# Fused attention and two feed-forward layers on one core: the first group's keys and values laid four tokens deep over 128 partitions

## What is computed

```
kv  = einsum('bhsd,bhse->bhde', k, v)          # 64 x 64 per head, a sum over 576 tokens
out = einsum('bhsd,bhde->bhse', q, kv)
x   = out / sqrt(mean(out*out, -1) + 1e-6) * g_norm   -> (2304, 512)
x   = silu(x @ w_in) @ w_out                    # layer 1, d_ff 2048
y   = ((x @ w_a) * (x @ w_b)) @ w_out2          # layer 2, d_ff 1536
```

## Time and profile before

| | |
|---|---|
| median of 3 runs | 872.2 us (870.73 to 873.78) |
| the profiled execution | 873.04 us |
| its span, first to last instruction | 871.2 us |
| mean granted TensorE clock | 0.998 |
| TensorE matmul busy | 860.4 us, 99% of the span |
| VectorE, ScalarE, GpSimd busy | 510.6, 279.0, 610.1 us |
| moved by DMA | 55.56 MB, mean 64 GB/s |

### The profile page before, as it was taken

One profiled execution on the slowest core, in us unless ns is written; L12 is line 12 of the kernel. 1 busy time (PEld: TensorE's weight loads), 2 busy tenths in 40 slices (PEclk: granted clock), 3 DMA queues, 4 the chain that ended last, 5 costly groups with the idle time before them and its releaser, 6 DMA issues.

```text
span 871.2 us, 16097 instructions
## 1 busy us (share of the span) xinstructions
PE 860.4 (99%) x6208; PEld 813.8 (93%) x6208; DVE 510.6 (59%) x776; ACT 279.0 (32%) x465; POOL 610.1 (70%) x889
## 2 busy tenths in 40 slices
PE   8899999999999999999999999999999999999998
PEld 5699999999999999999999999999999999999997
DVE  4665656757886666665765355364484553544636
ACT  3764434534543323222532122121242211212210
POOL 2566545666578777766778697797889876877760
PEclk9999999999999999999999999999999999999999
DMA  9664123111011111111101111021011330210104
GB/s 300 158 156 106 49 57 75 50 49 49 26 49 49 46 28 50 50 49 49 49 25 49 50 49 49 25 63 60 25 49 49 109 98 25 74 49 25 49 25 109
DMA packets 47002, 55.56 MB, mean 64 GB/s; under 512 B 11728, under 2 KB 32464, under 8 KB 46928
## 3 DMA queue, kind: packets, MB, share of 16 engines
q1 hardware_dynamic: 44192, 49.55, 19.9%
q10 hardware_dynamic: 2736, 4.98, 1.8%
HBM read 49.81 MB, written 4.72 MB: 63 GB/s over the span
## 4 chain that ended last, share of the span: by engine, by line
PE 98%; DVE 1%; issue 1%; ACT 0%; POOL 0%; POOLq 0%
PE ps L777 49%; PE ps L863 8%; PE ps L864 8%; PE ps L865 8%; PE ps L885 6%; PE ps L887 6%; PE ps L886 6%; PE ps L794 3%; PE ps L737 2%; PE ps L747 1%; PE ps L989 1%; PE ps L709 1%; PE ps L723 1%; DVE o_sb L1350 0%; DVE stat L1331 0%
## 5 line engine op out<-in xcount | busy, mean ns | idle before, releaser
L777 PE MATMUL ps<-x_hi,w_hi 128*128 128x288 f32 x1064 | 229.8, 297 | 0.5 <-issue 0.3
L777 PE MATMUL ps<-x_lo,w_hi 128*128 128x288 f32 x1064 | 228.1, 296 | 0.0
L777 PE MATMUL ps<-x_hi,w_lo 128*128 128x288 f32 x1064 | 226.8, 295 | 0.0
L777 PEld LDWEIGHTS ps<-x_hi,w_hi 128*128 128x128 f32 x1064 | 179.0, 188 | 13.7 <-issue 5.1
L777 PEld LDWEIGHTS ps<-x_hi,w_lo 128*128 128x128 f32 x1064 | 171.7, 189 | 0.0
L777 PEld LDWEIGHTS ps<-x_lo,w_hi 128*128 128x128 f32 x1064 | 169.9, 188 | 0.0
L1142 ACT COPY kept<-ps 128x576 f32<-128x576 f32 x114 | 73.2, 642 | 288.1 <-PE ps L777 287.6
L523 POOL TENSOR_SCALAR w_hi<-wt 128x256 fp32r<-128x256 f32 x152 | 69.9, 460 | 123.4 <-PE ps L777 116.4
L1473 DVE TENSOR_TENSOR xy<-xy,ps 128x384 f32<-128x384 f32 (+1 forms) x188 | 94.0, 510 | 89.0 <-PE ps L865 88.7
L863 PE MATMUL ps<-g_hi,d_hi 128*128 128x384 f32 x384 | 129.0, 336 | 0.2
L864 PE MATMUL ps<-g_lo,d_hi 128*128 128x384 f32 x384 | 128.9, 336 | 0.0
(11 more groups left out here) (111 smaller groups left out, 1236.7 us busy)
## 6 DMA issues: line engine op xcount, KB each, us to landing
raw<-in_moe_w_out_dram SPq DMA_DIRECT2D x28, 512.0 KB, 3.6
raw<-in_moe_w_in_dram SPq DMA_DIRECT2D x15, 512.0 KB, 3.5
raw<-in_moe_w_a_dram SPq DMA_DIRECT2D x12, 512.0 KB, 3.5
raw<-in_moe_w_b_dram SPq DMA_DIRECT2D x12, 512.0 KB, 3.5
kvq<-in_k_dram SPq DMA_DIRECT2D x8, 576.0 KB, 5.5
out_dram<-xy SPq DMA_DIRECT2D x26, 128.0 KB, 2.4
kvq<-in_v_dram ACTq DMA_DIRECT2D x4, 576.0 KB, 11.4
kvq<-in_v_dram SPq DMA_DIRECT2D x4, 576.0 KB, 5.9
```

The source lines that it names most:

```text
L777: mm = pe.matmul(ps[:, bank + s, 0:PART], w, x[:, n, c, s * PART:(s + 1) * PART], start=(begins and first), stop=last, skip_group_check=no ...
```

## The change

- Group 0's k and v: tokens 0 to 511 of a head are spread over all 128 partitions, four tokens deep (`main_heads`, one load for each batch: 256 pieces of 1 KB), and the last 64 tokens go, for the two heads, on 64 partitions each (`rest_heads`, one load for each head of k and of v: 128 pieces of 256 bytes). `kv(0, h)` is then 16 matmuls of 128 rows and 4 of 64 rows, where it was 36 of 64 rows.
- SyncE issues k, all rests and all of q; ScalarE issues v alone. SyncE also waits for the fourth `kv` before it loads group 1.
- Warm-up: 26 matmuls of 56 columns and 8 of 48, for 3 and 2 of 512.
- One order for all head pairs of group 0: `o_turn` of the pair before goes in turn with `q_kv`, and VectorE interleaves normalising and `qT_keep` from h = 0 on.
- Group 1's `kv_keep` copies first the bank that TensorE needs next and frees it with a semaphore of its own (`kv_first`).
- The last rest of segments 2 and 3 goes from GpSimd to VectorE (one instruction).
- The second half of the last down tile goes to `BANK_A`.

```diff
-    POOL_RESTS = (((0, 0), (0, 1), (7, 0), (7, 1), (5, 0), (5, 1)), (6,))
+    POOL_RESTS = (((0, 0), (0, 1), (7, 0), (7, 1), (5, 0), (5, 1)), (6,), (), ())
...
-    WARM = (3, 2)
+    WARM = ((26, 56), (8, 48))
...
+        def main_heads(h, which, bb):
+
+            dst = kvq[h][:, which, main_at(bb, 0, 0).start:main_at(bb, 1, DEEP - 1).stop].rearrange("p (h e) -> p h e", h=2)
+            return dst, (k, v)[which][bb, 2 * h:2 * h + 2, 0:MAIN].rearrange("h (p t) d -> p h (t d)", t=DEEP)
+
+        def rest_heads(h, which, odd):
+            dst = kvq[h][odd * HALF:(odd + 1) * HALF, which, rest_at(0).start:rest_at(1).stop]
+            return dst.rearrange("p (b d) -> p b d", b=2), (k, v)[which][0:2, 2 * h + odd, MAIN:].rearrange("b p d -> p b d")
...
-            return BANK_D + (tile_turn[DOWN0[-1] - 1] + c) % 2
+            return (tile_bank(DOWN0[-1] - 1), BANK_A)[c]
...
             for h in range(PAIRS):
-                sp.dma_start(*heads(0, h, 0)).then_inc(kv_in[h], 16)
-                sp.dma_start(*queries(h, 0)).then_inc(q_in[h], 16)
+                for bb in range(2):
+                    sp.dma_start(*main_heads(h, 0, bb)).then_inc(kv_in[h], 16)
+                for which in range(2):
+                    for odd in range(2):
+                        sp.dma_start(*rest_heads(h, which, odd)).then_inc(kv_in[h], 16)
+                for bb in range(2):
+                    sp.dma_start(*queries(h, bb)).then_inc(q_in[h], 16)
...
             sp.wait_ge(q_in[PAIRS - 1], 32)
+            sp.wait_ge(kv_mm, PAIRS)
             load_heads(0)
...
-                if u == PROD0[seg_of(pair_of(u))]:
-                    x_rest(seg_of(pair_of(u)), 6)
+                if u == PROD0[1]:
+                    x_rest(1, 6)
...
+                    for t in range(DEEP):
+                        for odd, bank in enumerate((b0, b1)):
+                            for bb in range(2):
+                                cols = main_at(bb, odd, t)
+                                pe.matmul(ps[bb * HALF:(bb + 1) * HALF, bank, 0:HD],
+                                          kvq[h][:, 0, cols], kvq[h][:, 1, cols], start=(t == 0), stop=False)
...
+                if G:
+                    turn[BANK_D + kv_order(G, h)[0]] = (kv_first, h + 1)
...
                 for j in range(JS):
-                    if h > 1:
+                    if h:
                         o_turn(0, h - 1, j, result_bank(h - 1, j))
                     q_kv(0, h, j, prod_bank(h, j))
...
             for h in range(PAIRS):
-                nc.scalar.dma_start(*heads(0, h, 1)).then_inc(kv_in[h], 16)
-                nc.scalar.dma_start(*queries(h, 1)).then_inc(q_in[h], 16)
+                for bb in range(2):
+                    nc.scalar.dma_start(*main_heads(h, 1, bb)).then_inc(kv_in[h], 16)
...
-                flush(3, 4)
+                flush(3, 3)
+                late_rest(pp, 6)
+                flush(4, 4)
```

More of the change, by code:

```diff
@@ L30, in fused_attention_ffn_kernel @@
     TILE3 = 3 * P
+    DEEP = SEQ // P
+    MAIN = DEEP * P
     JS = ROWS // 3
     UNITS = PAIRS * JS
-    assert KT == 4 and ROWS % 3 == 0 and SEQ == 2 * PART and PART <= 512
+    assert KT == 4 and ROWS % 3 == 0 and SEQ == 2 * PART and PART <= 512 and SEQ - MAIN == HALF
     SEGS = [(g, layer) for layer in (1, 2) for g in range(GROUPS)]
@@ L398, in x_split @@
         def x_split(seg, n, c=1):
[L400 to L405, removed]
+            what = n if seg else (n, c)
+            split, signal = (POOL_RESTS, side_ready) if what in POOL_RESTS[seg] else (DVE_RESTS, x_ready)
+            return signal, split[seg].index(what) + 1 + sum(len(rests) for rests in split[:seg])
         def temps(seg):
@@ L467, in load_heads @@
                 for which in range(2):
-                    sp.dma_start(*heads(1, h, which)).then_inc(kv_in[0], 16)
+                    sp.dma_start(*heads(h, which)).then_inc(kv_in[0], 16)
                 for bb in range(2):
@@ L703, in kv @@
                 wait_turn(b1)
-                for t in range(ROWS):
+                if G:
+                    for t in range(ROWS):
+                        for odd, bank in enumerate((b0, b1)):
+                            rows = slice(odd * HALF, odd * HALF + HD)
+                            for bb in range(2):
+                                cols = slice(bb * SEQ + t * HD, bb * SEQ + (t + 1) * HD)
+                                mm = pe.matmul(ps[bb * HALF:(bb + 1) * HALF, bank, 0:HD],
+                                               kvq[0][rows, 0, cols], kvq[0][rows, 1, cols],
+                                               start=(t == 0), stop=(t == ROWS - 1))
+                else:
+                    for t in range(DEEP):
+                        for odd, bank in enumerate((b0, b1)):
+                            for bb in range(2):
+                                cols = main_at(bb, odd, t)
+                                pe.matmul(ps[bb * HALF:(bb + 1) * HALF, bank, 0:HD],
+                                          kvq[h][:, 0, cols], kvq[h][:, 1, cols], start=(t == 0), stop=False)
                     for odd, bank in enumerate((b0, b1)):
-                        rows = slice(odd * HALF, odd * HALF + HD)
                         for bb in range(2):
-                            cols = slice(bb * SEQ + t * HD, bb * SEQ + (t + 1) * HD)
+                            rows, cols = slice(odd * HALF, (odd + 1) * HALF), rest_at(bb)
                             mm = pe.matmul(ps[bb * HALF:(bb + 1) * HALF, bank, 0:HD],
-                                           kvq[buf][rows, 0, cols], kvq[buf][rows, 1, cols],
-                                           start=(t == 0), stop=(t == ROWS - 1))
+                                           kvq[h][rows, 0, cols], kvq[h][rows, 1, cols], start=False, stop=True)
                 mm.then_inc(kv_mm, 1)
                 turn[b0] = turn[b1] = (kv_kept, PAIRS * G + h + 1)
+                if G:
+                    turn[BANK_D + kv_order(G, h)[0]] = (kv_first, h + 1)
             def q_turn(G, h, j, bank):
@@ L983, in layer2, with warm @@
                 down2(pp - 1, 8)
-            def warm(count):
+            def warm(count, cols):
                 for _ in range(count):
                     zeros = wt[:, 0:2, :].rearrange("p a n -> p (a n)")
-                    pe.matmul(ps[:, first_bank(1, 0), :], ident[:], zeros, start=True, stop=True)
+                    pe.matmul(ps[:, first_bank(1, 0), 0:cols], ident[:], zeros[:, 0:cols], start=True, stop=True)
             pe.wait_ge(consts, 3)
             pe.wait_ge(cleared, 1)
-            warm(WARM[0])
+            warm(*WARM[0])
             kv(0, 0)
-            warm(WARM[1])
+            warm(*WARM[1])
             for j in range(JS):
@@ L1070, in kv_keep @@
                 act.wait_ge(cleared, 2)
-                for odd, bank in enumerate((BANK_D, BANK_D + 1)):
+                for place, odd in enumerate(kv_order(G, h)):
                     if n == 0 and odd:
@@ L1076, in kv_keep @@
                     for bb in range(2):
-                        cp = nc.scalar.copy(kv_sb[rows, h % 2, bb, rows], ps[bb * HALF:(bb + 1) * HALF, bank, 0:HD])
+                        cp = nc.scalar.copy(kv_sb[rows, h % 2, bb, rows],
+                                            ps[bb * HALF:(bb + 1) * HALF, BANK_D + odd, 0:HD])
+                    if G and place == 0:
+                        cp.then_inc(kv_first, 1)
                 cp.then_inc(kv_kept, 1)
@@ L1689, in _ @@
                     normalise(0, h, j)
-                    if 0 < h < PAIRS - 1:
+                    if h < PAIRS - 1:
                         qT_keep(0, h + 1, j, first_bank(h + 1, j))
-                if h == 0:
-                    for j in range(JS):
-                        qT_keep(0, 1, j, first_bank(1, j))
             first_pair()
```

36 lines of the change are left out of this document (20 added, 16 removed).

## The result

The changed kernel takes 875.77 us in the median (875.45 to 876.86, 7 runs), the kernel before in the same comparison 872.34; the ratio is 1.0047, with a 95% interval of 1.0033 to 1.0061 (the quotient of the two medians is 1.0039). It is slower by 0.4 to 0.5%, where I had forecast 868.5 us. The span of the profiled execution is 874.5 us where it was 871.2, 3.3 us more. The profiled execution of the kernel before, 873.04 us, is one of its slower ones (its medians lie between 870.8 and 872.3), so a difference to that profile shows a loss about 1 us too small and a gain as much too large. One execution of e12 took 1403 us at a mean granted clock of 0.557; it is left out of that kernel's median and range.

The account below looks back on a forecast made before the run. Late TensorE code (two stalls) and the loads bound the head; after it TensorE is full. Gains of 1.8 (head), 0.9, 0.8 and 0.25 sum to 3.75 us: 869.3 profiled, 868.5 us median; range 865.7 to 872.0.

Parts of the forecast that it names:

- the lower end: First warm-up at the start: columns set the time, so 52 records of 56 columns take 5.2 us.
- upper end: First warm-up if each record costs as a 128-column one: it ends at 10.5 us, costing about 1 us.
- The loads: Head: new loads bring q of the four head pairs at 12.4, 19.4, 23.2 and 27.1 us, or up to 3 later.
- 1.9 lost by data: Head: later q makes the second head pair end at about 23.4 us, before 21.46; a loss of 1.9 us.
- The stalls for code: Head: two TensorE stalls are code late behind full data queues; their end, with the second's clock fall, wins 3.7 us.
- Rival A: Head: the stalls are not late code, so the mid-product one and its clock fall remain; 872.2 us, chance 0.10.
- The order: Head: with one order for all, head pairs 2 and 3 follow at 6.72 us each, ending at 30.1 and 36.8.
- The sums: `kv` matmuls of a head pair: 1.12 us, or 2.1 at most; lower end taken, as long as before, no gain.
- SyncE's issues: Head: 34 load issues at 0.64 us end near 22.5 us and do not set the time.
- rival D: Head: SyncE's many issues are slow, at 1.15 us each the last q is issued at 39.8; 876.7 us, chance 0.05.
- The late edits: After the head: group 1's banks 0.9, last rest on VectorE 0.8, last half tile's bank 0.25 us won.
- rival B: Head: the code packet waits longer, or gaps before 20 us lower the clock, costing 1.5 to 2 us; 870.2, chance 0.20.

Follow-up runs that it names:

- e12: The kernel of e2 timed again: changed kernel with old warm-up, old loads and old sums; 870.90 us, ratio 0.9996.
- e7: e2 with the second warm-up as 8 matmuls of 64 columns for 2 of 512, 24 instructions more; 868.72 us (one execution).
- e3: The kernel before with only the new warm-up; 877.73 us, ratio 1.0065.
- e1: The changed kernel with the old warm-up (3 and 2 matmuls of 512 columns); 871.82 us, ratio 0.9994.
- e10: The changed kernel with a long warm-up of 7 and 2 matmuls of 512 columns; 871.52 us, ratio 1.0001.
- e5: e1 with the rests of v and half of q moved to ScalarE's queue; 874.15 us, ratio 1.0026.
- e6: e5 with head pair 0 in the old layout and loads; 873.11 us, ratio 1.0015.
- e9: e6 with v alone on ScalarE from the second head pair on; 871.71 us, ratio 1.0007.
- e2: e1 with the old loads and 36-matmul sums; new order, hold of group 1's loads and late edits stay; 869.83 us, ratio 0.9984.
- e8: e2 without SyncE's wait that holds back group 1's loads; 872.37 us (one execution).
- e11: The kernel of e7 timed: e2 with 24 more instructions in the second warm-up; 868.64 us, ratio 0.9968.
- e4: The kernel before with only the three late edits (group 1's banks, last rest on VectorE, last bank); 869.18 us, ratio 0.9977.

## Why the prediction was wrong

**The warm-up: the step that failed.** The prediction took "the lower end", 5.2 us by columns, "and keep 1 in the range". It measured 11.34 us. Even its upper end had 10.5 with the last 29 records at full clock, because the clock had risen near 7 us before. It did not rise. The records show a pace of 218 ns throughout. The upper end had priced a record at 244 ns at the lower level and 122 at the full one, so its prices were about right, and only its clock was wrong. The narrow columns save nothing: a float32 record with 128 x 128 weights has a price that is not its 56 columns, and in the profile the weight loads fill the whole of that time. The clock column reads 1.00 in this stretch, as it did before for the first 7 us, so the level is read from the durations: 3.47 us for 36 records against 2.19, 228 ns against 125 for a like record in e7, 239 ns against 128 for a record of the first transposes. The price is not only the 5.9 us of the longer warm-up but also 1.3 us at the first `q_kv`, 1.7 at the second warm-up and 1 at the first transposes. e3 puts the whole at +4.5 us of head, +5.9 of time; e1 takes 4.0 off.

By the prediction's sum layer 1 starts at 36.7 us (38.5 - 1.8). It started at 43.31, 6.6 late: 5.1 of it is the warm-up (43.31 against 38.21 in e10, which differs in nothing else), and 1.5 is the loads. With the late edits 0.45 short of their sum this is the 7.05 us between the forecast span (871.2 - 3.75) and 874.5.

The Trainium skill ("TensorE: Matmul & The Clock Gate", The HAM clock gate) says that a busy array is granted 2.4 GHz and an idle one 1.2. The lower level after 3.4 us without work in e1 agrees. In after and e3 TensorE was busy for 11 us without a gap, with narrow matmuls, and the full clock did not come; here the measurement differs from that sentence. Why, no run here shows.

**The loads: mechanism right, size too small.** Forecast arrivals of q were 12.4, 19.4, 23.2 and 27.1 to 30; measured 13.70, 21.39, 26.93 and 31.92 (19.7 for the second in e1 and e10). The first sum's data came at 10.3 us in e1, at least 3.3 later than before; the prediction had not worked that out. The term "1.9 lost by data" is 4.0 us: in e10, without stall or low clock, the second head pair ends at 25.47, where the prediction had 23.4 and the kernel before 21.46. One term of the working was read too low. The 177 GB/s of the earlier trace rows hold some pieces of 2 KB among the 256-byte ones: 1,151 pieces in 2 us are 1.7 ns a piece, not 1.45. That is 0.15 us a head pair, too little to be the cause. The 0.33 us set against the 0.74 is the pace of the 2,304-byte pieces, 401 GB/s.

**The stalls for code: the mechanism right, the credit not shown.** No "issue" gap stands in the head of any kernel with the short code (after, e1, e5, e6, e9, e10). With the long code two came back (e2, e12), moved with the count of instructions (e7), and a third came when group 1 was not held (e8). In e2, e7, e8, e11 and e12 the packet of each stall begins 2.4 to 3.1 us before TensorE moves (read from windows of 0.25 us), as in the two of the earlier trace rows (2.5 to 2.9). Rival A is out. What is not shown is that the short code is what took the stalls away: e3 has the old code and no stall, only because TensorE comes later, and in each kernel with the short code TensorE is late too, for data or clock. No run has the short code with early data. The Trainium skill ("Runtime: NRT & Kernel Launch", Instruction fetch mechanics) calls the crossing mostly hidden. Behind full data queues it is not, with up to 2.3 us a crossing here (e8). Past the head it is: no wait of TensorE without a releaser is over 0.3 us in before and 0.2 in after.

**The order: right in pace.** Head pairs follow at 6.4 us (forecast 6.72). But e4 with the old order has 6.4 us from its third to its fourth pair as well (31.51 to 37.92); the 6.72 of the kernel before had the 0.3 us in it by which its 12 records at 34.79 were late. **The sums: right.** 1.31 us from start to start (30.40 to 31.71) against 1.2 before: no gain from half as many matmuls. **SyncE's issues**: to 24.85 instead of 22.5 us, rival D's beginning, but q was issued in time. **The late edits: right**, 1.5 to 1.65 of 1.95 us.

**The clock (rival B)** had its chance for "the longer gaps". In the kernel after the lower clock came, but not from gaps: the full clock was not reached before some 22 us. In e1, e5, e6 and e9 it came from gaps of 2.4 to 6.3 us as B had it. The forecast was on the wrong side since the sum took the warm-up at its lower end, and its upper end took over a rise of the clock that had been seen only behind the old, wide matmuls. Without that step it would still have been off: e10, whose warm-up is wide, is the same as before.

## What to carry to other kernels

A warm-up is part of the path when it is longer than the wait that it covers: size it by the measured time of one record, not by columns, use matmuls of a form that a trace has shown to bring the full clock (512 columns here), and see that the ordinary matmuls after it run at full pace. A gap on TensorE without a releaser in the midst of a product, one code packet behind it on the instruction queue, is code that came late behind data: move its boundary (fewer or more instructions ahead of it), or hold back loads that are not needed yet. Count the issues of loads on an engine that has other work: 21 on ScalarE held its first copy until 18.45 us. And a stall that moves with the number of instructions ahead of it can vanish by being reached later; to credit the shorter code, keep the arrival of the data the same.

## What the runs showed of the hardware that was not expected

- 52 records of 128 x 56 and 16 of 128 x 48 float32 matmuls without a gap run at 218 and 228 ns and leave TensorE at its lower clock past 20 us (after, e3); behind 6 records of 512 columns in 5.5 us it ran at the full one by 7 us (before).
- Behind the first stall the next code packet began 4.9 to 6.3 us after TensorE had moved again (before, e2, e4, e8, e12), while the head's loads filled the queues; behind the second, with group 1's loads held back, 1.7 to 2.6 us after (e2, e7, e11, e12). Kernels that stall range over 2.9 to 4.8 us in time (e11, e2), those that do not over 0.7 to 2.2 us (e10, e5), and e3, with the long code but no stall, over 1.0 in four runs.
- 24 more instructions near the start made the kernel 2.3 us faster (e11 against e12). The only other thing that differs between the two is what the second warm-up computes, at the same length; the first code packet began at 11.9 us instead of 16.9.
